# Pass 0's weight units are issued a round or a slot later: loads 1 to 7 of a fused attention and MLP kernel

## The reference

```python
def attention(q, k, v):              # each (4 batches, 8 heads, 576, 64)
    # branch 1: q, k, v averaged over groups of 4 positions, full softmax attention
    # on the 144 means, each output repeated 4 times
    # branch 2: softmax attention on positions with |i - j| < 4 only
    return out_up + out_local
x = attention(q, k, v) as (2304 tokens, 512)
g = x @ w_gate                        # 512 x 1536
x = (silu(g) * (x @ w_val)) @ w_out   # 1536 x 512
h = max(x @ w2_in, 0)                 # 512 x 2048
return (h * h) @ w2_out               # 2048 x 512
```

## Time and profile before

| | |
|---|---|
| Three runs, median (lowest, highest) | 901.86 us (901.82, 902.78) |
| The profiled execution, its own time | 902.37 us |
| Its span | 900.5 us, mean granted TensorE clock 1.0 |
| Busy: PE / DVE / ACT / POOL | 888.2 / 649.2 / 400.2 / 220.9 us |
| SP and ACT queues' DMA traffic | 65.55 MB and 4.72 MB |

### The profile page before, as it was taken

One profiled execution on the slowest core, in us unless ns is written; L12 is line 12 of the kernel. 1 busy time (PEld: TensorE's weight loads), 2 busy tenths in 40 slices (PEclk: granted clock), 3 DMA queues, 4 the chain that ended last, 5 costly groups with the idle time before them and its releaser, 6 DMA issues.

```text
span 900.5 us, 17396 instructions
## 1 busy us (share of the span) xinstructions
PE 888.2 (99%) x6794; PEld 866.0 (96%) x6794; DVE 649.2 (72%) x1113; ACT 400.2 (44%) x733; POOL 220.9 (25%) x278
## 2 busy tenths in 40 slices
PE   7999999999999999999999999999999999999998
PEld 5689999999999999999999999999999999999998
DVE  7886576662778575887575898585788575788784
ACT  3575555652455344645353544242535242435331
POOL 5866456543431001502001321000412000202000
PEclk9999999999999999999999999999999999999999
DMA  8883443222312021311312220010232020221422
GB/s 216 230 224 95 123 122 97 62 73 84 104 49 71 1 71 44 107 63 36 106 36 95 88 100 1 1 36 24 83 106 71 1 71 1 82 83 50 126 71 71
DMA packets 70881, 71.38 MB, mean 79 GB/s; under 512 B 27280, under 2 KB 58000, under 8 KB 70800
## 3 DMA queue, kind: packets, MB, share of 16 engines
q1 hardware_dynamic: 68496, 65.55, 24.4%
q10 hardware_dynamic: 2304, 4.72, 1.4%
HBM read 56.10 MB, written 14.16 MB: 78 GB/s over the span
## 4 chain that ended last, share of the span: by engine, by line
PE 89%; DVE 5%; ACT 2%; issue 2%; POOL 1%; DMA 0%; DVEq 0%; SPq 0%; ACTq 0%
PE mlp_ps L1050 12%; PE mlp_ps L1051 12%; PE mlp_ps L1052 12%; PE scores L1050 9%; PE scores L1051 9%; PE scores L1052 9%; PE xp L1051 4%; PE xp L1050 4%; PE xp L1052 4%; PE tr L1050 2%; PE tr L1051 2%; PE tr L1052 2%; PE tr L851 1%; PE xp L920 1%; PE xp L938 1%
## 5 line engine op out<-in xcount | busy, mean ns | idle before, releaser
L1484 ACT ACTIVATE wh_hi<-hbuf 128x384 fp32r<-128x384 f32 x144 | 70.8, 522 | 94.6 <-DVE hbuf L1795 69.2
L722 POOL TENSOR_TENSOR w_raw<-w_raw 128x256 f32<-128x256 f32 x16 | 14.1, 880 | 360.4 <-DMA w_raw<-w_in 360.4
L1803 DVE TENSOR_TENSOR wh_lo<-hbuf,wh_hi 128x384 fp32r<-128x384 f32 x144 | 76.5, 560 | 23.1 <-ACT wh_hi L1484 19.8
L1758 DVE TENSOR_TENSOR ring<-ring_raw,ring 128x768 fp32r<-128x768 f32 x96 | 91.5, 975 | 0.0
L1433 ACT ACTIVATE ring<-ring_raw 128x768 fp32r<-128x768 f32 x96 | 75.3, 836 | 28.8 <-DVE ring_raw L1752 28.5
L1050 PE MATMUL scores<-ring,w_hi 128*128 128x384 f32 x240 | 80.5, 335 | 0.2 <-ACT hbuf L1458 0.2
L1051 PE MATMUL scores<-ring,w_hi 128*128 128x384 f32 x240 | 80.2, 334 | 0.0
L1052 PE MATMUL scores<-ring,w_lo 128*128 128x384 f32 x240 | 80.2, 334 | 0.0
L1052 PE MATMUL mlp_ps<-ring,w_lo 128*128 128x384 f32 x240 | 80.2, 334 | 0.0
L1050 PE MATMUL mlp_ps<-ring,w_hi 128*128 128x384 f32 x240 | 80.2, 334 | 0.0
L1051 PE MATMUL mlp_ps<-ring,w_hi 128*128 128x384 f32 x240 | 80.2, 334 | 0.0
(11 more groups left out here) (211 smaller groups left out, 2529.0 us busy)
## 6 DMA issues: line engine op xcount, KB each, us to landing
ring_raw<-x_whole SPq DMA_DIRECT2D x24, 384.0 KB, 3.8
ring_raw<-y_whole SPq DMA_DIRECT2D x24, 384.0 KB, 3.4
qk_sb<-qT SPq DMA_DIRECT2D x16, 288.0 KB, 3.9
qk_sb<-kT SPq DMA_DIRECT2D x16, 288.0 KB, 5.1
v_grp<-v SPq DMA_DIRECT2D x32, 144.0 KB
x_whole<-x_f ACTq DMA_DIRECT2D x16, 288.0 KB, 2.5
y_whole<-ypart SPq DMA_DIRECT2D x3, 1536.0 KB, 5.7
v_win<-v SPq DMA_DIRECT2D x64, 64.0 KB, 3.1
```

Source lines behind the costliest of these rows:

```text
L722: nc.gpsimd.tensor_tensor(block(5), block(7), block(4), ALU.add).then_inc(s_usum[i], 1)
L1484: nc.scalar.activation(hi[:, f, t, :], hbuf[:, e, :], ACT.Copy).then_inc(s_shhi, 1)
L1758: nc.vector.tensor_tensor(ring[:, SLOTS[g][p], 1, :, :], whole(g, p), ring[:, SLOTS[g][p], 0, :, :].bitcast(F32), ALU.subtract).then_inc(s ...
L1803: nc.vector.tensor_tensor(lo[:, f, t, :], hbuf[:, e, :], hi[:, f, t, :].bitcast(F32), ALU.subtract)\
```

## The change

Only two tables change, and with them SP's order; no other engine's order differs.

```diff
-ROUND_LOAD = {0: [0], 1: [1], 2: [2], 3: [3], 4: [4, 5]}
-SLOT_LOAD = {0: [6, 7]}
+ROUND_LOAD = {0: [0], 2: [1], 3: [2], 4: [3, 4]}
+SLOT_LOAD = {0: [5], 1: [6, 7]}
 ROUND_HI = {1: [0], 3: [1], 4: [2]}
 SLOT_HI = {0: [3], 1: [4], 2: [5], 3: [6], 4: [7]}
```

## The result

The changed kernel took 903.85 us (median of 16 executions, 902.08 to 907.87), the kernel before 901.79 us (16 executions): ratio 1.0026, 95% interval 1.0017 to 1.0034. It is slower, by some 2.1 us between the medians; 904.4 was forecast, 901.9 to 906.2 the range.

What follows compares the result with a forecast made beforehand. PE bounds the kernel, so delays in the head are paid in full: +2.9 for ACT's two waits, -0.4 for the earlier `v_grp`, +2.5 on 902.37 makes 904.9, or 904.4 us for the median; range 901.9 to 906.2.

Steps and rivals of the forecast that it cites:

- The bound: PE is busy 888.2 of 900.5 us, so only the head counts and its delays are paid in full at the end.
- Unit 1, no cost: ACT's hi step: issued at 32.36, the unit lands at 36.66, just before ACT wants it at 36.73; cost nothing.
- Unit 2, a wait of 3.1 us: ACT's hi step: the unit lands at 46.56, ACT wants it at 43.47; PE then waits 1.8 us for silu 0's bank.
- Unit 3, a wait of 2.9 us: ACT's hi step: ACT wants the unit at 49.7, it lands at 52.6, delaying pair 5's transposes to 65.3.
- The first wait is swallowed: On ACT, unit 2's wait vanishes in unit 3's later one, so both together cost only 2.9 us.
- The sum: Whole kernel: +2.9 for ACT's two waits and -0.4 for the earlier `v_grp`, +2.5 us.
- The gain in the head, -0.4: SP's `v_grp` ahead of unit 2 lands sooner without unit 1's 512 KB: 0.4 us, bounds 0 and 2.0.
- the ring-order rule: DMA queue: descriptors are consumed in ring order, so a load behind `v_grp` takes nothing from it; gain 0, sum 2.9.
- Rival D: On PE: idle gaps of 1.8 and over 1 us in the head drop the clock to 1.2 GHz; 911 us, chance 0.03.

Runs made afterwards that it cites:

- the usual profile: The changed kernel, unaltered, run again and profiled in an execution of 903.28 us; median 903.37 us against 901.60, ratio 1.0018.
- the long one: The changed kernel, unaltered, in the execution of its first measurement that was profiled: 907.87 us.
- the second profile: The kernel before, unaltered, run again and profiled in an execution of 900.65 us; median 901.87 us against 901.72, ratio 1.0007.
- the fill: The kernel before with POOL doing unit 0's lo step twice and 16 more `pe_keep_busy` matmuls on PE ahead of round 4's scores: 905.70 us, ratio 1.0045.

## Why the prediction was right, and where not

*The bound.* Right: span less transposes of pair 5 is 838.06 to 838.33 us in the eight profiles of the table, so all that changed lies in the first 68 us. (The last slice of PE in the earlier trace rows is an 8 and not a 9; nothing hangs on it.)

*Unit 1, no cost.* Right in the time (ratio 0.9993 with it alone), wrong in the working: ACT waited for it 0.99 us in the usual profile, 1.72 with it alone moved and 3.33 in the long one, not 0, in place of idle time it had anyway. It landed 5.8 us after its issue in the usual profile where 4.3 was forecast, and the same text had called it likely to be quicker.

*Unit 2, a wait of 3.1 us.* Right in kind, too large: 1.32 us in the usual profile, 2.70 at most. Its 6.0 us to landing was one sample; here it was 4.8. The 1.8 us that PE was to wait for silu 0's bank was 0.16; with a wait of 2.70 for unit 2 it was 1.54, so the path is as forecast.

*Unit 3, a wait of 2.9 us.* Confirmed in size and path: 2.89, 2.96, 2.28 us, and from hi step 4 to the transposes 10.5 us, as in the earlier trace rows, in the usual profile and with unit 1 kept (63.31 - 52.79, 65.31 - 54.79). It stands elsewhere, though: the unit landed 5.2 us after its issue where 5.1 was forecast, but was issued at 45.50 and not 47.52, and taken at 50.72 and not 52.6.

*"The first wait is swallowed."* This step failed. It said that with or without unit 2's wait the cost was 2.9 us; with units 3 to 7 alone the medians differ by 1.1 us, and the ratio leaves at most 1.4. I had treated the places in SP's queue as fixed, and they are not: from round 3's `v_grp` to the next round's first unit it is 6.3 us in one profile and up to 8.2 in another. That they move with the bytes ahead is likely and not shown.

*The sum.* +2.5 forecast, 2.1 and 1.8 measured. Two terms were mis-sized and partly cancel: the base held a 2.32 us wait for unit 4 that the second profile does not have, and units 2 and 3 came sooner than their old places said. Against the profile that the sum started from, the transposes of the usual execution are 0.9 us later (63.31 against 62.40), not 2.5; against the second they are 2.5 later. That the forecast lies so near the medians is in part luck in which execution was profiled first.

*The gain in the head, -0.4.* Not shown: POOL's wait for the v groups of pair 2 was 2.40 and 1.39 us in the two profiles of before, 1.35 and 4.00 in those of the changed kernel. Over all fourteen profiles it averages 1.6 us in the eight with unit 1 in round 1 (0 to 2.40) and 2.0 in the six without (0.62 to 4.00), so no gain is seen. Within that spread the ring-order rule of the Trainium skill (DMA: Bandwidth & Descriptors, "Queues, rings and completion order"), from which I had worked out a gain of 0, is neither confirmed nor refuted.

*Rival D.* I gave it 0.03 and argued from the slices that a slice with PE 7 tenths busy kept its clock. In three of 16 executions, and two of 12 later, the time was 906.1 or more, and the one that was profiled had the clock at half. But the clock is not what makes an execution long: of these five, two (907.47 and 906.14) have a mean granted clock of 1.000, two 0.998 and only the profiled one 0.992; and the kernel before has executions at 0.996 too, none over 905.45. In the profiled one the place was another than I named, a wait for POOL near 36, not one for ACT near 50 (the fill's profile has one of that kind, 1.59 us near 56, and the clock fell behind it; in the usual profile, after 1.54 us, it did not); a 22.5 us slice says nothing on one gap of 2 us. The rule of the Trainium skill cited there (TensorE: Matmul & The Clock Gate, "HAM oscillation") agrees in kind with the rows of this run, 2.49 us idle and then 0.50. Its price was not mine: of the 4.5 us in span over the usual profile, 3.2 are there at hi step 4 already (55.94 against 52.79), and as much at the landing of unit 3, whose issue hangs on POOL's release; 1.5 us were added behind it.

*Open.* Why v groups issued at about 23 us land near 26 in one execution and near 30 in another. None of 122 executions of the kernel before was over 905.45, five of 28 of the changed one were at 906.1 or more; that the change makes them likelier is seen, by which path is not: two of the five are long with the clock full, and none of those was profiled.

## What to carry to other kernels

A load's slack is not the distance to its consumer in one trace: find the engine that would wait, what stands behind it on that engine, and what reserve the bottleneck has there, and move no load closer than its slowest landing seen. Where an issuing queue waits for another engine's release, every load behind that wait inherits its lateness (42.5 against 39.7 here); that making the other engine faster wins it back did not show, in an edit that also loaded a third engine. Profile twice before leaning on a wait of 2 us: here the same kernel had it once and once not.

## What was not expected of the hardware

The granted clock stayed at half for very different times after a gap of PE: some 13.7 us after 2.49 us idle, 3.4 us after 3.56, though PE was busy after it in both but for 0.5 us near 42. The same transfers landed at very different times from one execution to the next: POOL's wait for the v groups of pair 2 was 1.35 and 4.00 us in two executions of the changed kernel, and that difference alone is more than the 2.1 us of the change.
